# Eight pairs' x kept on chip until mixing, and the by-state rows laid where w_tok's first rows come

## What is computed

```
attention:  state = alpha[t] * state + k[t] (outer) v[t];   x[t] = q[t] @ state
mixing:     theta = x @ w_theta;  zr, zi = x*cos(theta), x*sin(theta)
            u0 = x + w_tok_r @ zr + w_tok_i @ zi            (w_tok: 768 x 768, over tokens)
            u  = u0 + relu(u0 @ w_ch)
gated FF:   h = relu(u @ w_in);  g = h * sigmoid(conv3(h));  y = g @ w_out
```

## Time and profile before

| what | us |
|---|---|
| median of 3 runs | 541.23 (541.16 to 541.58) |
| the profiled execution: its own time | 542.85 |
| its span (first to last instruction) | 541.1 |
| PE busy | 527.5 (97%) |
| DVE busy | 443.8 (82%) |
| ACT busy | 289.6 (54%) |
| POOL busy | 75.7 (14%) |
| DMA | 52.29 MB, mean 97 GB/s |

### The profile page before, as it was taken

How to read it: one execution, slowest core, us unless ns; L and a number is a source line. 1 busy time by engine, 2 the same in 40 slices (tenths; PEclk the granted TensorE clock), 3 DMA queues, 4 the chain that set the end, 5 groups by cost and what they waited for, 6 DMA issues and landing times.

```text
span 541.1 us, 11731 instructions
## 1 busy us (share of the span) xinstructions
PE 527.5 (97%) x4116; PEld 519.9 (96%) x4116; DVE 443.8 (82%) x799; ACT 289.6 (54%) x609; POOL 75.7 (14%) x70
## 2 busy tenths in 40 slices
PE   5899999999999999999999999999999999999997
PEld 5899888899999999999999999999999999999997
DVE  7899977799987677866696777899798989889884
ACT  5788776865643443444344553455464454546353
POOL 7788777000000000000000000000000000000000
PEclk9899999999999999999999999999999999999999
DMA  8999997374303020211035002202020202101011
GB/s 205 262 275 254 289 264 230 116 232 147 113 1 117 21 63 17 102 29 50 33 93 188 13 6 85 88 2 87 1 88 0 87 22 66 60 27 44 1 45 44
DMA packets 34363, 52.29 MB, mean 97 GB/s; under 512 B 3632, under 2 KB 24496, under 8 KB 34320
## 3 DMA queue, kind: packets, MB, share of 16 engines
q1 hardware_dynamic: 31504, 47.69, 29.7%
q10 hardware_dynamic: 2816, 4.03, 2.2%
HBM read 37.55 MB, written 14.16 MB: 96 GB/s over the span
## 4 chain that ended last, share of the span: by engine, by line
PE 94%; DMA 2%; DVE 1%; POOL 1%; issue 1%; SPq 0%; ACT 0%; ACTq 0%; POOLq 0%
PE y_bank L1436 28%; PE y_bank L1495 19%; PE theta_bank L1482 9%; PE x_bank L1482 9%; PE theta_bank L1423 7%; PE y_bank L1466 7%; PE weighed L1340 4%; PE x_sum L1305 3%; PE x_sum L1318 3%; PE turned L1327 2%; PE x_bank L1411 1%; DMA x_in<-x_scratch 1%; DMA a_in<-in_a_rows 1%; PE turned L1345 1%; DVE before L1104 0%
## 5 line engine op out<-in xcount | busy, mean ns | idle before, releaser
L1495 PE MATMUL y_bank<-first_w,z 128*128 128x384 f32 x576 | 109.8, 336 | 0.0
L1495 PEld LDWEIGHTS y_bank<-first_w,z 128*128 128x128 f32 x576 | 101.0, 188 | 0.0
L1436 PE MATMUL y_bank<-first_w,z 128*128 128x384 f32 x432 | 78.7, 340 | 0.1
L1436 PE MATMUL y_bank<-rest_w,z 128*128 128x384 f32 x432 | 76.8, 337 | 0.0
L1436 PEld LDWEIGHTS y_bank<-first_w,z 128*128 128x128 f32 x432 | 75.1, 188 | 0.3 <-issue 0.3
L1436 PEld LDWEIGHTS y_bank<-rest_w,z 128*128 128x128 f32 x432 | 74.6, 188 | 0.0
L1255 DVE TENSOR_SCALAR x_rows<-out_rows,taps 128x384 f32<-128x384 f32 x64 | 26.9, 420 | 19.8 <-ACT out_rows L1021 19.6
L1021 ACT ACTIVATE out_rows<-theta_bank 128x386 f32<-128x386 f32 x32 | 15.8, 493 | 51.1 <-PE theta_bank L1482 51.1
L1423 PE MATMUL theta_bank<-theta_w,x_t 128*128 128x384 f32 x216 | 41.8, 338 | 0.0
L1262 DVE SCALAR_TENSOR_TENSOR z_full<-out_rows,taps,x_rows 128x384 f32<-128x384 f32 x64 | 39.6, 620 | 2.2
L1258 DVE SCALAR_TENSOR_TENSOR x_rows<-out_rows,taps,x_rows 128x384 f32<-128x384 f32 x64 | 39.6, 618 | 2.3
(11 more groups left out here) (129 smaller groups left out, 986.8 us busy)
## 6 DMA issues: line engine op xcount, KB each, us to landing
v_in<-in_v_tokens SPq DMA_DIRECT2D x16, 288.0 KB, 5.1
x_in<-x_scratch SPq DMA_DIRECT2D x24, 192.0 KB, 2.5
a_in<-in_a_rows SPq DMA_DIRECT2D x30, 146.2 KB, 5.0
k_in<-in_k_rows SPq DMA_DIRECT2D x30, 144.0 KB, 4.9
q_in<-in_q_rows SPq DMA_DIRECT2D x30, 144.0 KB, 4.8
y<-x_all SPq DMA_DIRECT2D x7, 576.0 KB, 3.3
x_scratch<-x_rows SPq DMA_DIRECT2D x26, 144.0 KB, 3.7
u_scratch<-u_sum ACTq DMA_DIRECT2D x6, 576.0 KB, 3.5
```

Source lines behind the costliest of these rows:

```text
L1436: ins = pe.matmul(y_bank[2 * d + half][:, 0:HALF], z[s % 2][part][zp][:, d * P:(d + 1) * P], mixing_w(part, wp, s)[:, half_tokens(half)], ...
L1495: ins = pe.matmul(out_bank[half][t][:, 0:MODEL], g[k % 4][gp][:, t * P:(t + 1) * P], out_w[wp][f], start=f == 0 and i == 0, stop=f == FF_T ...
```

## The change

Pairs 5 to 12, not 10 to 12, are kept on chip. The five new row buffers lie in `late_places`, in the space of `rest_w` (tiles 4 and 5: pieces 8 to 11). The by-state rows move from there to the space of `first_w` (pieces 0 to 5). The late stores are made in two parts: pairs 5, 6, 7 in mixing step 0 and pairs 8 to 12 in mixing step 1, each part with a semaphore of its own. ACT waits for the first before `high(8)` and for the second before `high(10)`; SP waits for the first (and for pair 4's store) before it loads tile 0 of batch 1. DVE computes one more spare batch number, and SP reads two numbers, not one, ahead of the late stores. `x_scratch` has one spare batch more.

```diff
-KEPT_LATE = (10, 11, 12)
+KEPT_LATE = (5, 6, 7, 8, 9, 10, 11, 12)
+
+STORED_LATE = {0: (5, 6, 7), 1: (8, 9, 10, 11, 12)}
...
                 do.load_weight(s)
-                if s == 1:
-                    do.store_late()
+                if s in STORED_LATE:
+                    do.store_late(s)
...
     with ExitStack() as own:
-        x_late = ring("x_late", len(KEPT_LATE), [P, SEQ], on=own)
+        x_late = ring("x_late", 3, [P, SEQ], on=own)
     channel_w = ring("channel_w", 2, [P, MODEL_TILES, MODEL], F32R)
+    with ExitStack() as own:
+        by_state = StateByState(nc, own, ctx)
     first_w = [ring(f"first_w{part}", 2, [P, FIRST_TILES, SEQ], F32R) for part in range(2)]
     with ExitStack() as own:
-        by_state = StateByState(nc, own, ctx)
+
+        late_places = sb("late_places", [P, 8 * SEQ], F32, own)
+        x_late = [late_places[:, u * SEQ:(u + 1) * SEQ] for u in (1, 4, 7, 2, 5)] + x_late
         kept_raw = ring("kept_raw", 3, [P, SEQ], on=own)
...
+    def all_stored_late(eng, s):
+        eng.wait_ge(late_stored[s], 32 * len(STORED_LATE[s]))
...
         def decide():
-            sp.wait_ge(judged, 4)
+            sp.wait_ge(judged, 5)
             by_state.if_out_of_range(sp, in_range, by_state.path_sync(a_rows, k_rows, q_rows, v_rows, x_scratch, x_stored))
-            to_batch[LAST] = sp.value_load(x_batch[0:1, 0:1], min_val=LAST, max_val=BATCH)
+            to_batch[LAST] = sp.value_load(batch_of[LAST][0:1, 0:1], min_val=LAST, max_val=BATCH)
...
-        def store_late():
-            to_batch[LAST - 1] = sp.value_load(late_batch[0:1, 0:1], min_val=LAST - 1, max_val=BATCH + 1)
-            for o in KEPT_LATE:
+        def store_late(s):
+            if s == 0:
+                for b in (LAST - 1, LAST - 2):
+                    to_batch[b] = sp.value_load(batch_of[b][0:1, 0:1], min_val=b, max_val=BATCH + LAST - b)
+            for o in STORED_LATE[s]:
                 x_copied.done(sp, 2 * o + 1)
-                store_rows(o, late_stored)
+                store_rows(o, late_stored[s])
...
         def load(b, s):
+            if isinstance(b, int) and b == 1 and s == 0:
+                x_stored[0].done(sp, 2)
+                all_stored_late(sp, 0)
...
         def spare(b):
             if isinstance(b, int):
-                sp.wait_ge(late_stored, 32 * len(KEPT_LATE))
+                all_stored_late(sp, 1)
...
-            if n == len(pieces) - 1:
-                act.wait_ge(late_stored, 32 * len(KEPT_LATE))
+
+            if n == 2 * (TOKEN_TILES - 2):
+                all_stored_late(act, 0)
+            if n == 2 * (TOKEN_TILES - 1):
+                all_stored_late(act, 1)
             act.activation(pieces[n].high, raw_of(n), ACT.Copy).then_inc(piece_high.sem, 1)
...
         def place():
-            dve.tensor_scalar(x_batch[:, :], total[:, :], 0.0, float(LAST), ALU.is_gt, ALU.add).then_inc(judged, 1)
+            dve.tensor_scalar(batch_of[LAST][:, :], total[:, :], 0.0, float(LAST), ALU.is_gt, ALU.add).then_inc(judged, 1)
             dve.wait_ge(judged, 3)
 
-            dve.tensor_scalar(late_batch[:, :], x_batch[:, :], 3.0, float(-2 * LAST - 1), ALU.mult, ALU.add).then_inc(judged, 1)
+            for back, b in ((1, LAST - 1), (2, LAST - 2)):
+                dve.tensor_scalar(batch_of[b][:, :], batch_of[LAST][:, :], float(2 * back + 1), float(b - (2 * back + 1) * LAST),
+                                  ALU.mult, ALU.add).then_inc(judged, 1)
```

More of the change, by code:

```diff
@@ L454, in layer @@
     unused, quarter, least, most = (sb(x, [P, 1]) for x in ("unused", "quarter", "least", "most"))
-    in_range, x_batch, late_batch = (sb(x, [1, 1], mybir.dt.int32) for x in ("in_range", "x_batch", "late_batch"))
+    in_range = sb("in_range", [1, 1], mybir.dt.int32)
+    batch_of = {b: sb(f"batch_of{b}", [1, 1], mybir.dt.int32) for b in range(1, BATCH)}
     x_tokens = ring("x_tokens", 2, [P, MODEL])
@@ L571, in layer @@
     piece_high, piece_low = count("piece_high"), count("piece_low")
-    late_stored, one, pads, later_pads, const, dve_const, pool_const, all_measured, judged = (
-        signal("att_" + x) for x in ("late_stored", "one", "pads", "later_pads", "const", "dve_const", "pool_const", "all_measured", "judged"))
+    late_stored = [signal(f"att_late_stored{s}") for s in STORED_LATE]
+    one, pads, later_pads, const, dve_const, pool_const, all_measured, judged = (
+        signal("att_" + x) for x in ("one", "pads", "later_pads", "const", "dve_const", "pool_const", "all_measured", "judged"))
     theta_got, theta_high_done, theta_low_done = (signal("att_theta_" + x) for x in ("got", "high", "low"))
@@ L1139, in divert @@
         def divert():
-            dve.wait_ge(judged, 4)
+            dve.wait_ge(judged, 5)
             by_state.if_out_of_range(dve, in_range, by_state.path_vector(ident))
@@ L1512, in build @@
           moe2_w_in, taps, moe2_w_out, y):
-    x_scratch = nc.dram_tensor("x_scratch", (BATCH + 2, MODEL, SEQ), F32).ap()
+    x_scratch = nc.dram_tensor("x_scratch", (BATCH + 3, MODEL, SEQ), F32).ap()
     u_scratch = nc.dram_tensor("u_scratch", (BATCH, P, MODEL_TILES, SEQ), F32).ap()
```

## The result

The changed kernel takes 539.58 us in the median (538.33 to 541.88, 15 runs), the kernel before 541.58 (539.98 to 544.78, 15 runs): a ratio of 0.9963, with a 95% interval of 0.995 to 0.9976. That is 2.0 us less, between 1.3 and 2.7; 538.9 had been forecast, a gain of 2.3. The size is near. Its make-up, as the experiments show, is not: about half of it or more comes from a place that the forecast had priced at nothing.

A forecast was written before the change was run, and what follows sets the result against it. PE, busy for 97% of the span, was taken as the bound. The profiled 542.85 us less 2.28 (1.12 + 1.02 + 0.14) is 540.57; the median stands 1.62 lower, giving 538.95, taken as 538.9, range 538.1 to 541.0.

The forecast's parts named there:

- The bound: Whole kernel: PE is busy for 97% of the span, so only its standstills or the time before its unbroken run can gain.
- From there on nothing is gained: From mixing on, PE is busy 10.00 of 10 us; moving transfers gains nothing, the end moves only with mixing's start.
- Stores out of steps 7 to 11: Attention: removing the stores of pairs 5 to 9 lets the DMA queue drain; 1.12 + 1.02 + 0.14 = 2.28 us gained.
- The holes at 63.99 and 71.05: PE's two gaps in attention steps 10 and 11, 1.12 and 1.02 us, both taken to go entirely.
- The second hole as a late fetch: Gap at 71.05: PE ran out of instructions whose fetch came late behind data; all 1.02 us gained, bounds all or nothing.
- The tail: End of attention: PE's 0.33 us wait for ACT's k_tokens, ACT being held by x tile 0; none taken as gain.
- The extra DVE instruction: One more in step 14, 0.14 us, covered by PE's 0.33 us wait: cost 0, or 0.14 without that cover.
- Mixing: Stores added in mixing steps 0 and 1: 5.3 MB at 273 GB/s ends at 128.0, covered by 1 us; cost 0.
- Places of buffers: The buffers' new places move no transfer and no instruction: 0.
- Only the q load's hole goes: Rival, attention: the fetch's hole has another cause and stays; gain 1.26, time 540.0 us; chance 0.15.
- Given back: Rival, before mixing: ACT waits longer at x tile 0's load by what the steps saved; 541.2 us; chance 0.12.
- slower: Rival, first mixing steps: the queue backs up, pieces 8 and 9 and tile 5 land late; 544.0 us at 190 GB/s; chance 0.11.

The follow-up runs named there:

- pad_only: The kernel before plus one unused one-element tile ahead of x_tokens, nothing else: 540.67 us, ratio 0.9977 to the kernel before.
- after_third: The changed kernel, unaltered, timed again on the same chip as three other kernels: 539.56 us, ratio 0.9963 to the kernel before.
- unpad_after: The changed kernel plus one more unused one-element tile, which puts z at 130976: 540.82 us, ratio 0.9981 to the kernel before.
- before_again: The kernel before, unchanged, run and traced again: 541.98 us, ratio 1.0017 to itself.
- mix_only: The kernel before plus ten more 144 KB stores in mixing steps 0 and 1, attention's stores left in: 542.11 us, ratio 1.0013.
- layout_only: The changed kernel with its places, waits and small instructions, but only pairs 10 to 12 kept, other stores back in attention: 540.03 us, ratio 0.9978.
- copy_more: The kernel before with the unused tile, plus a 295 kB DRAM copy beside each store of pairs 5 to 9: 543.40 us, ratio 1.0037.
- double_late: The changed kernel plus sixteen more stores in mixing steps 0 and 1, 32 in all: 550.57 us, ratio 1.0171 to the kernel before.

## Why the prediction was right, and where it was not

**The bound.** PE bounds the attention steps and the rest gains only by starting sooner: right for attention. "From there on nothing is gained" is true of transfers, and failed for the whole change, since the run of PE itself became 1.0 us shorter.

**Stores out of steps 7 to 11: 2.28 us.** The direction and the cause hold. Bytes, not issues: taking them away while keeping SP's issues keeps the gain (539.73 against 539.95), and adding as many again costs 2.7 us, with POOL waiting for q. The size was too large by a factor of two to three. With equal places of buffers, on one chip, `pad_only` and `after_third` stand at 540.67 and 539.56: 1.1 us, or 0.8 by the two ratios, whose intervals overlap. All kernels with the change's places of buffers say the same: ratios of 0.9977 and 0.9978 with the stores in attention, and of 0.9963, 0.9963, 0.9967 and 0.9968 without, 0.7 us in the mean. `unpad_after` is 0.4 us under the kernel before in the medians and 1.0 by its ratio, but its places differ, and 0.2 us of that are theirs (434.5 against 434.7). The step that failed is the reading of one trace. The holes at 63.99 and 71.05 were priced as if they stood in every execution, and `before_again` and `mix_only`, with no hole over 0.7 us there, are 2 us faster in these steps. Nor are steps 2 to 6 free of holes, as the forecast took it from its trace: `before_again` has one of 0.56 us in step 3. That the profiled execution was 1.6 us over the median stood in the forecast's own sum, and should have been taken as a sign of it.

**The second hole as a late fetch.** It was neither proved nor refuted. A hole inside a run of PE's own work, with no semaphore, was found again in `pad_only`, twice (1.57 and 1.09 us). It wasn't found in any of the traces with pairs 5 to 9 kept, nor in those of `before_again`, `mix_only`, `layout_only` and `copy_more`, which store them in attention. The one at 71.24 stands again behind a long stretch without an instruction block. `pad_only`'s DMA queues from 60.5 to 69.6 us, with no line for the instruction queue:

```profile
q1 hardware_dynamic: 984, 2.21, 104.0%
issues: line engine op xcount, KB each, median us to landing
```

In `pad_only` the blocks before that hole came 11 us apart, and before, 9.9; in the other traces the longest distances between 40 and 85 us are 6.7 to 8.9 (9.5 in `copy_more`), with no such hole; `copy_more` has a wait of 0.40 us near there, at 84.9, but its row names ACT's copy of x. So far the fetch fits. But the second hole of `pad_only`, at 79.50, stands behind blocks only 8.1 us apart, so the distance alone doesn't decide. The three holes do go with a block: each begins 1.5 to 1.6 us after a block's fetch has begun (at 69.46 before, at 69.77 and 77.89 in `pad_only`). But those fetches take 1.2, 1.6 and 1.1 us, so in two of the three cases the block was there 0.4 to 0.5 us before the hole began. The Trainium skill (DMA: Bandwidth & Descriptors, Queues, rings and completion order) says that each DMA engine goes round the queue rows that have work, packet by packet. No run here changed the fetch by itself, so neither that rule nor the forecast's reading is tested, and the cause of these holes stays open.

**The tail.** The forecast took none of the 0.33 us at x tile 0, as nothing near it is removed. In the traces the stretch from step 15 to mixing is 0.28 shorter on average and never over 16.52 with the stores out. PE's wait for k_tokens there (0.33, 0.25 and 0.16 us) is found in three of the five traces with them in, and in none without, so that term is there in some executions. The extra DVE instruction is hidden, as forecast.

**Mixing.** It was priced at 0, and 0 is what the trace of `mix_only` shows. The bytes were over-priced and the issuing under-priced: the first mixing steps moved 343 GB/s where 273 was assumed, but a store took SP 0.60 us in the changed kernel's step 0 (3.61 / 6) and 0.82 in `double_late`, where 0.485 was assumed, and in `double_late` the first thing late is the x tile.

**Places of buffers: 0.** This is the term that was missing. "The new places of buffers move no transfer and no instruction" is true and not enough: an unused tile of 32 bytes gives 1.0 us of trace and 0.3 to 2.2 us in the timed ratio. So 538.9 was near 539.58 by luck: a term too large by 1.2 to 1.6 stood beside one too small by 1.0.

**The rivals.** "Only the q load's hole goes" has 1.26 us, near what the stores are worth, but for another reason. "Given back" and "slower" did not happen; `double_late` shows that the slower one is real: it comes somewhere between 16 and 32 stores.

## What to carry to other kernels

Before a stall in one trace is priced, compare the profiled execution with the median, and take a second trace of the same kernel: stalls that come from a crowded DMA queue move about, and only their mean is there to be gained. When a change adds or drops a small tile, look at where the big matmul operands begin afterwards, and time the old kernel with a dummy tile beside the new one. To tell bytes from issues, keep the issue and shrink the transfer.

## What the runs showed of the hardware

- Where buffers begin changes PE's rate. With z at byte 130912 of a partition (and the x_t, u_part and in_w buffers at the same remainder, 96 of 128) mixing takes 220.40 us. At 130944 and 130976 it takes 219.7. The FF stage takes 214.3 to 214.4, 213.9 to 214.0 and 214.8 at the three. The difference is spread over hundreds of matmuls, with no wait. Why, and which of the buffers does it, no run shows.
- The DMA share in the windows is no measure of room. It was 1.01 to 1.03 at 244, 262 and 291 GB/s alike.
- PE's granted clock before the steady steps differs from trace to trace: from 18 to 22 us it was 0.65 to 1.00, and step 2 took 5.18 us at 1.00 and 6.46 at 0.67.
- A fuller queue costs the issuing engine too: 0.82 us for a store in `double_late` against 0.485 in the kernel before.
